# One ScalarE queue, two neighbouring steps exchanged: the rounding of an earlier unit ahead of the arctangent

## The chip, the cores and the metric

The kernel runs on one core of one Trainium2 chip. The metric is the device time of one execution in microseconds. Three runs of the kernel before gave 1058.86 to 1060.13 us, with a median of 1059.6 us.

## The reference

Three things are computed one after the other, all in float32. The first is a gated linear attention over 4 batches of 8 heads, 768 tokens and 48 values a head. Its output, regrouped to 3072 tokens of 384 features, goes through a first feed-forward stage with 2048 hidden units and the Mish function, and the result goes through a second one with 1536 hidden units and a sigmoid gate.

```python
def _attn_ref(q, k, v, f_logit):
    f = 1.0 / (1.0 + np.exp(-f_logit))
    for t in range(S):
        state = f[:, :, t, :, None] * state + np.einsum('bhd,bhe->bhde', k[:, :, t], v[:, :, t])
        y[:, :, t] = np.einsum('bhd,bhde->bhe', q[:, :, t], state)

def _moe_ref(x, w_in, w_out):
    h = x @ w_in
    sp = np.where(h > 20.0, h, np.log1p(np.exp(np.minimum(h, 20.0))))
    return (h * np.tanh(sp)) @ w_out

def _moe2_ref(x, w_gate, w_val, w_out):
    gate = 1.0 / (1.0 + np.exp(-(x @ w_gate)))
    return (gate * (x @ w_val)) @ w_out
```

## The kernel before, in words

The program has three stages. Attention runs from 0 to about 189.6 us of the span, the first feed-forward stage (Mish) from there to about 605 us, and the second one to the end. Each engine has its own hand-written queue, and semaphores join them. An engine works its queue strictly in the written order. The change is in the Mish stage alone, so the rest of this section is about it.

The 3072 tokens are taken in three passes (NPASS) of 1024 tokens. A pass is two tiles (TP) of 512 tokens. The 2048 hidden units are 16 blocks of 128. A **unit** i of a pass is one block with one tile, so a pass has N1 = 32 units, i = 0 to 31. A pass takes 33 steps (POS1), one per unit and an empty one at its end, because three buffer sets (NSET) are used in turn.

All matmuls are float32 products in three parts (high times high, high times low, low times high), which is what the helper `three` issues. So each matrix that feeds one is split into a rounded high part and a remainder.

For unit i the work is this, with the name of the function, the line and the engine:

- `hidden` (L841 to L843, TensorE): nine matmuls of 512 columns give the hidden values h(i) in one of two PSUM banks.
- `start` (L472, ScalarE): tanh of h/2.
- `silu` (L695, VectorE): a product with h, which also frees the PSUM bank.
- `angle` (L478, ScalarE): arctangent of the tanh. It waits on `tanh_done`.
- `square` (L484) and `shifted` (L490), ScalarE: two Square activations, each waiting for the one before it.
- `cubic` (L701) and `finish` (L708), VectorE: two products that end the Mish value g(i).
- `high` (L495, ScalarE): rounds g(i) to the high part `ghi`. It waits on `g_done`, which `finish` sets, and on `acc_done`, for a free buffer.
- `low` (L713, VectorE): the remainder `glo`.
- `project` (L841 to L843 with `ghi` and `glo`, TensorE): nine matmuls that add the unit to the sums in PSUM. It waits on `g_ready`, which `low` sets.

The queues are skewed against one another. In step i TensorE does `hidden` of unit i and then `project` of unit i-2 (LOOK = 2). ScalarE does `start`, `angle`, `square` and `shifted` of unit i and `high` of unit i-1. VectorE does `silu` of unit i, `low` of unit i-1, then `cubic` and `finish` of unit i. In the empty step TensorE has `project` of unit 30 straight behind that of unit 29, and ScalarE has only `high` of unit 31. In the first two steps of the next pass the sums are read out of PSUM: `sums_high` (L502, ScalarE, three copies) and `sums_low` (L721, VectorE, three subtractions).

GpSimd splits weights (L364 a cast, L366 a subtraction, both on 128x384 tiles). In the third pass it splits the weights of the next stage into the space of those just used: after `project` of every second unit it has two weight units to split, so four instructions in a row.

Of the kernel before, what the change touches and what calls it, by code (L numbers as in the profile page):

```python
# [81 lines left out]
def attention_mlp_mlp(nc, q, k, f, v, w_in, w_out1, w_gate, w_val, w_out2, out):  # L82
    with ExitStack() as ctx:
# [126 lines left out]
        def lag_b(p, i, lag):  # L210
            at = back(p, i, lag, POS1, NPASS)
            return at if at and at[1] < N1 else None
# [181 lines left out]
        def _(act):  # L394
# [102 lines left out]
            def sums_high(p, i):  # L497

                t = i - (N1 - TP)
                act.wait_ge(acc_done, p * N1 + i + 1)  # L500
                for c in range(KC):
                    act.activation(xhi[:, c, bass.ds(p * PASS + t * TILE, TILE)], acc[t * KC + c][:, :],  # L502
                                   ACT.Copy).then_inc(x2hi_done, 1)

            def mish(p, i):
                if (at := lag_b(p, i, LOOK + 1)) and at[1] >= N1 - TP:
                    sums_high(*at)
                for lag, do in ((0, start), (0, angle), (1, high), (0, square), (0, shifted)):
                    if at := lag_b(p, i, lag):
                        do(*at)  # L510

            run(act, NPASS, POS1, LOOK + 1, LOOK + 1, mish)


# [436 lines left out]
```

## Time and profile before

| what | value |
|---|---|
| median of three runs | 1059.6 us |
| the profiled execution | 1059.6 us, with a span of 1057.6 us |
| TensorE matmul, busy | 1015.0 us (96%) |
| TensorE weight load, busy | 824.8 us (78%) |
| VectorE, busy | 552.2 us (52%) |
| ScalarE, busy | 541.1 us (51%) |
| GpSimd, busy | 132.3 us (13%) |
| mean granted TensorE clock | 0.993 of 2.4 GHz |
| chain that ended last, by engine | PE 81%, DVE 10%, issue 5%, ACT 3% |

In the profile PE is TensorE, PEld its weight loads, DVE VectorE, ACT ScalarE and POOL GpSimd. Busy time is a share of the whole span. The Mish stage takes about 415 us of it, with 192 groups of nine matmuls on TensorE. A matmul's record is longer than the distance to the next one, since they are pipelined: the distance between two starts is what counts. An idle time is the gap on an engine just before an instruction, with the name of what ended it.

### The profile page before, as it was taken

What the parts mean: (1) busy time and instruction counts of PE and PEld (TensorE: products, weight loads), DVE (VectorE), ACT (ScalarE), POOL (GpSimd) and SP (SyncE); (2) the same over time, 40 slices, a digit from 0 to 9 for tenths busy, and PEclk for the clock granted to TensorE, in tenths of its full rate; (3) what the DMA queues carried; (4) which work ended last, traced back from release to release, by engine and by line L of the source; (5) the groups of instructions that cost most, each with busy time, mean ns of one, the idle gap of its engine ahead of it and who ended that gap; (6) DMA issues with size and microseconds to landing.
All of it is one profiled execution on the core that took longest, in us unless ns stands there. A gap on an engine that the chain in (4) does not pass through costs nothing.

```text
span 1057.6 us, 14107 instructions
## 1 busy us (share of the span) xinstructions
PE 1015.0 (96%) x4765; PEld 824.8 (78%) x4765; DVE 552.2 (52%) x843; ACT 541.1 (51%) x969; POOL 132.3 (13%) x147
## 2 busy tenths in 40 slices
PE   4999999899999999999999899999999999999997
PEld 3777777688887888878888688888888888888885
DVE  6999998566667666667777622222222222222221
ACT  5677776577777777787777622121321122321212
POOL 2222212500000000004455420000000000000000
PEclk9999999899999999999999999999999999999999
DMA  5444442200000000001111100000100000100001
GB/s 149 143 140 132 140 138 78 60 1 1 1 1 1 0 0 0 0 0 43 48 45 46 46 22 2 0 1 1 60 0 0 0 0 0 60 0 1 1 1 60
DMA packets 35339, 37.54 MB, mean 35 GB/s; under 512 B 4064, under 2 KB 26080, under 8 KB 35296
## 3 DMA queue, kind: packets, MB, share of 16 engines
q1 hardware_dynamic: 35296, 36.98, 11.7%
q8 instruction: 25, 0.41, 0.2%
q14 instruction: 18, 0.15, 0.0%
HBM read 32.24 MB, written 4.72 MB: 35 GB/s over the span
## 4 chain that ended last, share of the span: by engine, by line
PE 81%; DVE 10%; issue 5%; ACT 3%; DVEq 0%; DMA 0%; SPq 0%; ACTq 0%
PE bank L841 26%; PE bank L843 26%; PE bank L842 26%; DVE prefix L576 2%; DVE probs L603 1%; ACT qt L412 1%; DVE suffix L578 1%; DVE state L620 1%; DVE xlo L627 1%; PE bank L784 1%; PE bank L761 1%; DVE state L614 1%; DVE kb L592 1%; DVE qb L589 1%; PE bank L779 1%
## 5 line engine op out<-in xcount | busy, mean ns | idle before, releaser
L841 PE MATMUL bank<-xhi,whi 128*128 (+1 forms) x720 | 285.0, 396 | 4.2 <-DVE xlo L721 2.6
L843 PE MATMUL bank<-xhi,wlo 128*128 (+1 forms) x720 | 283.7, 394 | 0.0
L842 PE MATMUL bank<-xlo,whi 128*128 (+1 forms) x720 | 281.0, 390 | 0.0
L841 PE MATMUL bank<-ghi,whi 128*128 128x512 f32 x504 | 200.4, 398 | 8.1 <-DVE glo L713 7.8
L741 DVE TENSOR_TENSOR prod<-prod,bank 128x512 f32<-128x512 f32 x72 | 49.5, 688 | 290.2 <-PE bank L843 290.2
L843 PE MATMUL bank<-ghi,wlo 128*128 128x512 f32 x504 | 198.2, 393 | 0.0
L842 PE MATMUL bank<-glo,whi 128*128 128x512 f32 x504 | 197.0, 391 | 0.0
L841 PEld LDWEIGHTS bank<-xhi,whi 128*128 128x128 f32 x720 | 135.5, 188 | 33.6 <-DVE xlo L721 3.0
L843 PEld LDWEIGHTS bank<-xhi,wlo 128*128 128x128 f32 x720 | 135.4, 188 | 32.3
L842 PEld LDWEIGHTS bank<-xlo,whi 128*128 128x128 f32 x720 | 135.7, 188 | 31.0
L521 ACT ACTIVATE prod<-bank 128x512 f32<-128x512 f32 x72 | 43.2, 600 | 188.0 <-PE bank L843 188.0
L526 ACT ACTIVATE ghi<-prod 128x512 fp32r<-128x512 f32 x72 | 45.5, 632 | 155.4 <-DVE prod L741 155.4
L841 PEld LDWEIGHTS bank<-ghi,whi 128*128 128x128 f32 x504 | 95.0, 189 | 31.7 <-issue 6.5
L843 PEld LDWEIGHTS bank<-ghi,wlo 128*128 128x128 f32 x504 | 95.0, 188 | 22.7
L842 PEld LDWEIGHTS bank<-glo,whi 128*128 128x128 f32 x504 | 95.1, 189 | 21.1
L701 DVE SCALAR_TENSOR_TENSOR sets<-sets 128x512 f32<-128x512 f32 x96 | 77.5, 807 | 64.8 <-ACT sets L490 64.6
L472 ACT ACTIVATE sets<-bank 128x512 f32<-128x512 f32 x96 | 57.4, 598 | 82.6 <-PE bank L843 82.6
L713 DVE TENSOR_TENSOR glo<-sets,ghi 128x512 fp32r<-128x512 f32 x96 | 67.1, 699 | 45.0 <-ACT ghi L495 43.2
L412 ACT ACTIVATE qt<-qb,rtotal 64x128 f32<-64x128 f32 x192 | 76.6, 399 | 21.2 <-DVE rtotal L587 14.7
L761 PE MATMUL bank<-qt,kb 128*128 128x256 f32 x192 | 64.8, 436 | 23.2 <-ACT qt L412 15.4
L364 POOL CAST whi<-raw 128x384 fp32r<-128x384 f32 x44 | 36.3, 825 | 350.4 <-PE bank L843 336.6
L743 DVE TENSOR_TENSOR glo<-prod,ghi 128x512 fp32r<-128x512 f32 x72 | 50.8, 705 | 50.8 <-ACT ghi L526 50.8
(70 smaller groups left out, 1060.3 us busy)
## 6 DMA issues: line engine op xcount, KB each, us to landing
raw<-w_out_dram SPq DMA_DIRECT2D x28, 192.0 KB, 2.4
xb<-f_dram SPq DMA_DIRECT2D x48, 96.0 KB, 2.4
kb<-k_dram SPq DMA_DIRECT2D x48, 96.0 KB, 2.2
qb<-q_dram SPq DMA_DIRECT2D x48, 96.0 KB, 2.2
vb<-v_dram SPq DMA_DIRECT2D x24, 192.0 KB, 2.4
out_dram<-rows_out SPq DMA_DIRECT2D x18, 256.0 KB, 2.2
raw<-w_in_dram SPq DMA_DIRECT2D x16, 192.0 KB, 2.6
raw<-w_gate_dram SPq DMA_DIRECT2D x12, 192.0 KB, 2.5
```

The lines of the kernel that those rows point to most:

```text
L412: ins = act.activation(qt[rows, a, par, :], qb[rows, n % NCH, a, :], ACT.Copy, scale=rtotal[rows, n % 2, a:a + 1])
L472: act.activation(st[:, 0], h_ps[i % 2][:, :], ACT.Tanh, scale=0.5).then_inc(tanh_done, 1)
L521: act.activation(prod[:, i % NSET], h_ps[0][:, :], ACT.Sigmoid).then_inc(sig_done, 1)
L526: act.activation(ghi[:, i % 2], prod[:, i % NSET], ACT.Copy).then_inc(phi_done, 1)
L701: dve.scalar_tensor_tensor(st[:, 3], st[:, 3], Z_SHIFT, st[:, 2], ALU.add, ALU.mult).then_inc(cubic_done, 1)
L713: dve.tensor_tensor(glo[:, i % 2], sets[:, i % NSET, 1], ghi[:, i % 2].bitcast(F32), ALU.subtract).then_inc(g_ready, 1)
L741: dve.tensor_tensor(prod[:, i % NSET], prod[:, i % NSET], h_ps[1][:, :], ALU.mult).then_inc(p_done, 1)
L743: dve.tensor_tensor(glo[:, i % 2], prod[:, i % NSET], ghi[:, i % 2].bitcast(F32), ALU.subtract).then_inc(p_ready, 1)
L761: mm = pe.matmul(s_ps[a // 2][:, (a % 2) * 2 * C:(a % 2 + 1) * 2 * C], kb[:, n % 3, a, :], qt[:, a, :, :].rearrange("p h t -> p (h t)"), s ...
L841: pe.matmul(ps, hi, xh, start=first, stop=False)
L842: pe.matmul(ps, hi, xl, start=False, stop=False)
L843: return pe.matmul(ps, lo, xh, start=False, stop=last)
```

## The change

The order of five steps in ScalarE's queue is altered. `high` of the unit before stood behind `angle` of the present unit; now it stands ahead of it, right behind `start`. No instruction is added or removed, and no wait is altered. The queues of the other engines are the same.

```diff
@@ -505,7 +505,7 @@
             def mish(p, i):
                 if (at := lag_b(p, i, LOOK + 1)) and at[1] >= N1 - TP:
                     sums_high(*at)
-                for lag, do in ((0, start), (0, angle), (1, high), (0, square), (0, shifted)):
+                for lag, do in ((0, start), (1, high), (0, angle), (0, square), (0, shifted)):
                     if at := lag_b(p, i, lag):
                         do(*at)
```

On ScalarE in the middle of a pass, the queue from the last step of one unit into the next unit and the one after it was this before (`sets` are the three buffer sets, `bank` is PSUM with the hidden values, and `ghi` takes the rounded value of the unit before):

```order
L490 ACTIVATE sets<-sets,consts 128x512
L472 ACTIVATE sets<-bank 128x512
L478 ACTIVATE sets<-sets,consts 128x512
L495 ACTIVATE ghi<-sets 128x512
L484 ACTIVATE sets<-sets,consts 128x512
L490 ACTIVATE sets<-sets,consts 128x512
L472 ACTIVATE sets<-bank 128x512
L478 ACTIVATE sets<-sets,consts 128x512
```

At the same place on ScalarE it is now this:

```order
L490 ACTIVATE sets<-sets,consts 128x512
L472 ACTIVATE sets<-bank 128x512
L495 ACTIVATE ghi<-sets 128x512
L478 ACTIVATE sets<-sets,consts 128x512
L484 ACTIVATE sets<-sets,consts 128x512
L490 ACTIVATE sets<-sets,consts 128x512
L472 ACTIVATE sets<-bank 128x512
L495 ACTIVATE ghi<-sets 128x512
```

L495 has moved up by one row, so L478, L484 and L490 of the present unit all stand behind it now, where only L484 and L490 did.

The second place is ScalarE at the end of a pass, with unit 31, the empty step and the first copy of the sums. Before (the numbers tell PSUM banks and tensors apart; ISA is a wait):

```order
L472 ACTIVATE sets_75<-bank7 128x512
L478 ACTIVATE sets_75<-sets_75,consts_54 128x512
L495 ACTIVATE ghi_73<-sets_75 128x512
L484 ACTIVATE sets_75<-sets_75,consts_54 128x512
L490 ACTIVATE sets_75<-sets_75,consts_54 128x512
L495 ACTIVATE ghi_73<-sets_75 128x512
L502 ISA
L502 ACTIVATE xhi_51<-bank0 128x512
```

And now, on ScalarE at the same end of a pass:

```order
L472 ACTIVATE sets_75<-bank7 128x512
L495 ACTIVATE ghi_73<-sets_75 128x512
L478 ACTIVATE sets_75<-sets_75,consts_54 128x512
L484 ACTIVATE sets_75<-sets_75,consts_54 128x512
L490 ACTIVATE sets_75<-sets_75,consts_54 128x512
L495 ACTIVATE ghi_73<-sets_75 128x512
L502 ISA
L502 ACTIVATE xhi_51<-bank0 128x512
```

The first L495 is that of unit 30 and the second that of unit 31. Two instructions stood between them, and now three do.

## Rows read from the trace of the kernel before

**Rows 1.** Waits of all engines: waiting < waited for, us in total, times, longest.

```profile
DVE sets L701 <- ACT sets L490: 64.6, 92, 1.6
...
ACT sets L472 <- PE bank L843: 82.6, 90, 4.9
...
ACT ghi L495 <- DVE sets L708: 8.4, 7, 2.3
PE bank L841 <- DVE glo L713: 7.8, 6, 2.7
```

**Rows 2.** Timeline of a middle step: start us, duration us, instruction, idle before.

```profile
314.21 0.60 ACT L472 ACTIVATE sets<-bank 128x512 f32<-128x512 f32 x1 [0.90 <-PE bank L843]
...
314.85 0.73 ACT L478 ACTIVATE sets<-sets,consts 128x512 f32<-128x512 f32 x1
...
315.48 0.61 ACT L495 ACTIVATE ghi<-sets 128x512 fp32r<-128x512 f32 x1
...
316.00 0.71 ACT L484 ACTIVATE sets<-sets,consts 128x512 f32<-128x512 f32 x1
...
316.74 0.72 ACT L490 ACTIVATE sets<-sets,consts 128x512 f32<-128x512 f32 x1
...
317.50 0.69 DVE L701 SCALAR_TENSOR_TENSOR sets<-sets 128x512 f32<-128x512 f32 x1 [0.68 <-ACT sets L490]
...
318.16 0.40 PE L841 MATMUL bank<-ghi,whi 128*128 128x512 f32 x1
...
318.29 0.69 DVE L708 SCALAR_TENSOR_TENSOR sets<-sets 128x512 f32<-128x512 f32 x1
318.36 0.60 ACT L472 ACTIVATE sets<-bank 128x512 f32<-128x512 f32 x1 [0.90 <-PE bank L843]
```

**Rows 3.** Timeline at the end of the first pass, units 30 and 31.

```profile
323.77 0.61 ACT L495 ACTIVATE ghi<-sets 128x512 fp32r<-128x512 f32 x1
...
324.42 0.69 DVE L713 TENSOR_TENSOR glo<-sets,ghi 128x512 fp32r<-128x512 f32 x1 [0.59 <-ACT ghi L495]
...
325.16 0.50 PE L841 MATMUL bank<-ghi,whi 128*128 128x512 f32 x1 [0.62 <-DVE glo L713]
...
326.58 0.69 DVE L708 SCALAR_TENSOR_TENSOR sets<-sets 128x512 f32<-128x512 f32 x1
...
327.31 0.63 ACT L495 ACTIVATE ghi<-sets 128x512 fp32r<-128x512 f32 x1 [1.56 <-DVE sets L708]
```

**Rows 4.** Timeline of ScalarE, first unit of the third pass.

```profile
465.34 0.60 ACT L472 ACTIVATE sets<-bank 128x512 f32<-128x512 f32 x1 [0.28 <-PE bank L843]
465.97 0.72 ACT L478 ACTIVATE sets<-sets,consts 128x512 f32<-128x512 f32 x1
466.73 0.72 ACT L484 ACTIVATE sets<-sets,consts 128x512 f32<-128x512 f32 x1
```

**Rows 5.** Timeline: `high` early in each pass, `project` of unit 30.

```profile
203.21 0.63 ACT L495 ACTIVATE ghi<-sets 128x512 fp32r<-128x512 f32 x1 [1.08 <-DVE sets L708]
...
343.11 0.63 ACT L495 ACTIVATE ghi<-sets 128x512 fp32r<-128x512 f32 x1
...
460.82 0.50 PE L841 MATMUL bank<-ghi,whi 128*128 128x512 f32 x1 [0.62 <-DVE glo L713]
...
478.74 0.63 ACT L495 ACTIVATE ghi<-sets 128x512 fp32r<-128x512 f32 x1
...
596.53 0.47 PE L841 MATMUL bank<-ghi,whi 128*128 128x512 f32 x1 [0.72 <-DVE glo L713]
```

**Rows 6.** Timeline of the third pass, VectorE beside GpSimd.

```profile
588.54 1.02 POOL L366 TENSOR_TENSOR wlo<-raw,whi 128x384 fp32r<-128x384 f32 x1
...
588.78 1.33 DVE L701 SCALAR_TENSOR_TENSOR sets<-sets 128x512 f32<-128x512 f32 x1 [0.68 <-ACT sets L490]
...
590.21 0.81 DVE L708 SCALAR_TENSOR_TENSOR sets<-sets 128x512 f32<-128x512 f32 x1
```

**Rows 7.** Windows: stretch, busy us of each engine (instructions), granted clock, DMA.

```profile
200.00:204.00 4.00, 3.59 (x9) 2.89 (x10) 3.14 (x5) 2.86 (x6) 3.84 (x4) 0.57 0.34 98
```

## The prediction

> **What bounds the kernel now.** I read the waits first, then the timeline of one middle step, then the ends of the passes. In the middle of a pass TensorE waits for nothing: one step takes 318.36 - 314.21 = 4.15 us [rows 2], which is 18 matmuls at 0.23 us. ScalarE waits about 0.90 us for it in each step [rows 1, 2]. TensorE waits for the Mish value only 6 times in the whole stage, 7.8 us in total [rows 1], among them 0.62, 0.62 and 0.72 us ahead of `project` of unit 30 in the three passes [rows 3, 5]. So TensorE sets the pace, and the other engines have slack. The question is whether they still have it after the change.
>
> The number that decides this is not ScalarE's busy time (about 3.4 us of work in 4.15). It is a loop: `finish` of unit i-1 releases `high` of unit i-1. Whatever stands behind `high` in ScalarE's queue and leads to `finish` of unit i is in a chain that feeds itself once per unit. If one turn of it takes over 4.15 us, it, and not TensorE, sets the pace.
>
> **The loop before.** Each link is a distance between two starts:
> - `high` to `square`: 316.00 - 315.48 = 0.52 us [rows 2]
> - `square` to `shifted`: 316.74 - 316.00 = 0.74 [rows 2]
> - `shifted` to `cubic`: 317.50 - 316.74 = 0.76 [rows 2]
> - `cubic` to `finish`: 318.29 - 317.50 = 0.79, with rounding 0.80 in other steps; I take 0.80 [rows 2]
> - `finish` to the next `high`, where `high` is waiting: 327.31 - 326.58 = 0.73 [rows 3]
>
> The sum is 3.55 us, and the trace has it as such once, where TensorE does not hold it: 327.31 - 323.77 = 3.54 [rows 3]. That is 0.60 us under TensorE's 4.15, so the loop is hidden.
>
> **The loop after.** `angle` joins it. `high` to `angle` takes 0.52 us; the trace before has `high` ahead of `square` only, but neither follower depends on `high`, so I take the same value. `angle` to `square` is now bare, since nothing stands between them: 466.73 - 465.97 = 0.76 where that was so already [rows 4], against the 1.15 us that spanned a `high` before. I take 0.75, the 0.72 of the instruction and 0.03 for the semaphore. The turn is 0.52 + 0.75 + 0.74 + 0.76 + 0.80 + 0.73 = 4.30 us. The bounds of the new link are 0.52 + 0.63 (if `square` could follow without the wait's gap, as `angle` is followed by `high` now) and 0.63 + 0.76 (if `angle` followed `high` as `high` follows `angle` now), so 4.18 to 4.42 us for a turn. All are above 4.15. `start` is not in the loop: it is issued while VectorE does `cubic` and `finish`, which take 0.76 + 0.80 + 0.73 = 2.29 us from `shifted`, and `start` needs 0.63 + 0.51 of them. `silu` and `low` fit into the rest of VectorE's turn.
>
> **How it spends the slack.** At first `high` comes earlier: in that middle step 0.66 us after `start` (318.29 + 0.73 - 318.36) and not 1.27 [rows 2]. From `high` to its `project` it takes 325.16 - 323.77 = 1.39 us [rows 3]. In the middle step the value was there at 315.48 + 1.39 = 316.87, and `project` began at 318.16 [rows 2], so 1.29 us of slack. A loss of 0.15 us per unit eats this and the early gain in 9 to 13 units. From there each `project` waits, and at unit 30, which has no `hidden` ahead of it, the wait is about 2.1 us in place of 0.6. So the end of a pass follows from counting turns:
>
> - **First pass.** `high` of unit 1 is at 203.21 [rows 5], and by the new loop no sooner. 29 turns later, plus 1.39, `project` of unit 30 starts at 203.21 + 124.70 + 1.39 = 329.30. Before: 325.16 [rows 3]. That is +4.14 us.
> - **Second pass.** The first units are held by VectorE's `sums_low`, which the change leaves alone; `high` of unit 2 at 343.11 [rows 5] keeps its place in the pass. 343.11 + 28 x 4.30 + 1.39 = 464.90 against 460.82 [rows 5]: +4.08 us.
> - **Third pass, without GpSimd.** 478.74 + 120.40 + 1.39 = 600.53 against 596.53 [rows 5]: +4.00 us.
> - **GpSimd in the third pass.** Its splits of the next stage's weights run beside this. A `cubic` that begins inside L366 takes 1.33 us and not 0.69, and the `finish` behind it 0.81 [rows 6]. Before, that fell into the slack of 0.60 us of the loop. Now there is none and it adds in full. There are 14 such bursts from unit 1 to unit 27. The bursts start behind `project` of an odd unit, some 3.8 us after its `high` (1.39, then nine matmuls and the release), and last about 4.2 us, so with the new turn the `cubic` of the second unit after it, at 4.30 + 2.77 us, meets the last L366. Bounds: 0, if the new phase misses them; 0.64 + 0.12 + about a quarter more, so 1.0 us each, if a whole L366 is waited for. I take 0.64, the row's value for one caught `cubic`: 14 x 0.64 = +9.0 us.
> - **Between passes, twice.** `high` of unit 31 comes one new turn after that of unit 30, 4.30 and not 3.54 us. ScalarE had 0.28 us to spare ahead of `start` of the next unit 0 [rows 4]; the rest, 0.48, moves the next pass: +0.9 us for two. The end of the third pass is covered: TensorE does the first eighteen matmuls of the next stage there.
>
> Attention and the last stage do not move. Nothing in the queues of DMA, VectorE and TensorE is reordered; the stores and loads follow their consumers.
>
> Sum: 4.1 + 4.1 + 4.0 + 9.0 + 0.9 = 22.1 us. The profiled execution took 1059.6 us (its span 1057.6, 2.0 us around it), which is also the median, so the forecast is 1082 us, +2.1%.
>
> On the GpSimd term there is a rule. The row shows `cubic` begun 0.24 us after the start of a 1.02 us L366 and lengthened by 0.64 us [rows 6]. The Trainium skill (SBUF — State Buffer, "SBUF: two separate sides") says that VectorE and GpSimd share a pair of ports as an exclusive lock; a VectorE instruction with two SBUF inputs, against a GpSimd one that reads SBUF, blocks for the whole of the other. By that rule the loss depends on where in L366 the operation falls, and rises to a full L366, about 1.0 us, at the worst phase; the sum would be 14 x 1.0 = 14 us for this term and 1087 us in all. The trace agrees with the lock (588.54 + 1.02 = 589.56, and the 1.33 us end 0.55 us after it), and it speaks against this change, since a longer loop is exposed to every such block.
>
> **The rivals.**
> 1. *The loop misses GpSimd's bursts.* For: the phase of VectorE against `project` changes. Against: a burst takes some 4.2 us of every two turns, so a VectorE operation of the loop can hardly avoid it. 4.1 + 4.1 + 4.0 + 0.9 = 13.1 us: 1072.7 us.
> 2. *The bursts catch more*, two operations or a whole L366 each: 14 us, in all 27 us: 1087 us.
> 3. *Not slower: the earlier `high` is all that is seen.* The place is the wait ahead of `project` of unit 30. If the new turn takes under 4.15 us, nothing accumulates, and `high` of unit 30 is earlier by up to 1.27 - 0.66 = 0.61 us, so three waits of 0.62, 0.62 and 0.72 us shrink to almost nothing: -1.8 us, 1057.8 us. It decides from the point where `angle` and `square` together take under 1.12 us behind `high`, against my 1.27. Against it is that the second depends on the first, whose record alone is 0.72 us.
> 4. *The clock falls.* From 200 to 204 us, behind the one wait of 2.7 us [rows 1], the granted clock is 0.57, near the lower of its two levels, 1.2 and 2.4 GHz [rows 7]. The new waits of about 2.1 us at unit 30 could do so again. Nine matmuls fill 3.6 us of that stretch in place of 9 x 0.23 = 2.1, so 1.5 us each for up to three, and three more at unit 0: +9 us, 1091 us.
>
> **How the numbers follow.** Forecast 62% (own range 1077 to 1085), rival 1 15%, rival 2 12%, rival 4 5%, rival 3 6%. The range that holds 8 in 10 runs from 1071, which takes in rival 1, to 1087, rival 2. Within 0.2% (2.1 us) is what measurement cannot tell from no change. Slower by more is all but rival 3: 94%. Rival 3 is mostly within the bound: 4% same, 2% faster.
>
> **What the profile after would show.** In the middle of a pass from unit 13 on, `high` to `high` and `project` to `project` are 4.30 us apart and not 4.15, in the third pass 4.6 on average. `high` waits for `finish` in nearly every step, so L495 behind L708 rises from 7 waits to about 90 and to some 80 us, while ScalarE's 82.6 us of waiting for TensorE at L472 mostly go. TensorE's waits behind L713 become some 60, and about 2 us at unit 30. The third pass is longer by 13 us or so, the other two by 4 to 5. If the step stays at 4.15 us, the loop is wrong; if the third pass grows like the others, the GpSimd term is; if the matmul distance rises above 0.23 us, it is the clock.

## The result

| | before | after |
|---|---|---|
| median | 1059.87 us (1058.86 to 1060.62, 4 runs) | 1086.32 us (1085.74 to 1086.52, 4 runs) |
| profiled execution | 1059.6 us, span 1057.6 | 1084.98 us, span 1083.0 |

The ratio is 1.0249, with a 95% interval of 1.0231 to 1.0267: slower by 2.5%, where 2.1% was forecast (1082 us, range 1071 to 1087).

The waits of the profile after, in the columns of [rows 1], and next to the lines that stood there:

```profile
DVE sets L701 <- ACT sets L490: 123.7, 92, 1.6
ACT ghi L495 <- DVE sets L708: 109.1, 94, 2.1
...
PE bank L841 <- DVE glo L713: 19.1, 20, 2.6
...
ACT sets L472 <- PE bank L843: 8.1, 7, 5.4
```

The relation has turned round. ScalarE waited 82.6 us for TensorE before and waits 8.1 us now; `high` waited for `finish` 7 times and does so 94 times out of 96, for 109.1 us. ScalarE and VectorE have become a ring of two engines waiting for each other, at 50% and 51% busy. Busy shares alone would not name them as the bound. The chain that ended last says it in one line (share of the span by engine; before it was PE 81%, DVE 10%, ACT 3%):

```profile
PE 46%; ACT 25%; DVE 21%; issue 6%; DVEq 1%; DMA 0%; SPq 0%; ACTq 0%
```

One turn of the ring in the middle of the first pass, on ScalarE, in the timeline after (start, duration, idle before):

```profile
315.56 0.63 ACT L495 ACTIVATE ghi<-sets 128x512 fp32r<-128x512 f32 x1 [1.07 <-DVE sets L708]
316.10 0.71 ACT L478 ACTIVATE sets<-sets,consts 128x512 f32<-128x512 f32 x1
316.84 0.72 ACT L484 ACTIVATE sets<-sets,consts 128x512 f32<-128x512 f32 x1
317.60 0.72 ACT L490 ACTIVATE sets<-sets,consts 128x512 f32<-128x512 f32 x1
318.23 0.58 ACT L472 ACTIVATE sets<-bank 128x512 f32<-128x512 f32 x1
319.88 0.63 ACT L495 ACTIVATE ghi<-sets 128x512 fp32r<-128x512 f32 x1 [1.07 <-DVE sets L708]
```

and its two links on VectorE:

```profile
318.36 0.69 DVE L701 SCALAR_TENSOR_TENSOR sets<-sets 128x512 f32<-128x512 f32 x1 [1.44 <-ACT sets L490]
319.15 0.69 DVE L708 SCALAR_TENSOR_TENSOR sets<-sets 128x512 f32<-128x512 f32 x1
```

319.88 - 315.56 = 4.32 us a turn, against TensorE's 4.15 [rows 2]. The links are 0.54, 0.74, 0.76, 0.76, 0.79 and 0.73. `start` (L472) stands in the hole ahead of `high` and costs nothing, as reckoned.

TensorE now takes its pace from the ring. `project` follows `hidden` at 0.33 and 0.31 us where two matmuls are 0.23 us apart otherwise, and one `project` starts 4.32 us behind the other (312.75 and 317.07 us):

```profile
312.42 0.39 PE L843 MATMUL bank<-xhi,wlo 128*128 x1
312.75 0.47 PE L841 MATMUL bank<-ghi,whi 128*128 128x512 f32 x1
313.06 0.40 PE L842 MATMUL bank<-glo,whi 128*128 128x512 f32 x1
```

Such a hold is shorter than the overlap of two matmul records, so the list of waits leaves it out: of TensorE's 20 waits for `low` none lies in the middle of the first two passes.

In the third pass GpSimd's splits come beside it. VectorE, then GpSimd, after:

```profile
500.16 1.31 DVE L713 TENSOR_TENSOR glo<-sets,ghi 128x512 fp32r<-128x512 f32 x1
502.29 1.19 DVE L701 SCALAR_TENSOR_TENSOR sets<-sets 128x512 f32<-128x512 f32 x1 [0.82 <-ACT sets L490]
503.59 0.69 DVE L708 SCALAR_TENSOR_TENSOR sets<-sets 128x512 f32<-128x512 f32 x1
```

```profile
499.91 1.02 POOL L366 TENSOR_TENSOR wlo<-raw,whi 128x384 fp32r<-128x384 f32 x1
500.87 0.97 POOL L364 CAST whi<-raw 128x384 fp32r<-128x384 f32 x1
501.92 1.02 POOL L366 TENSOR_TENSOR wlo<-raw,whi 128x384 fp32r<-128x384 f32 x1
```

`cubic` (L701) begins inside the second L366 and takes 1.19 us, not 0.69. 501.92 + 1.02 = 502.94, and `cubic` ends 0.54 us behind that. Every second turn is 4.82 us, the others 4.32.

Where the 25.4 us between the two profiled executions are, from the starts of `high` (L495) of units 2 and 30 in each pass (the Mish stage ends at 607.67 us before and 633.01 after, where TensorE's first matmul of the last stage starts):

| stretch | before | after | difference | forecast |
|---|---|---|---|---|
| start to `high` 30, first pass | 323.77 | 328.50 | +4.73 | +4.14 |
| to `high` 2, second pass | 19.34 | 19.69 | +0.35 | +0.48 |
| to `high` 30, second pass | 116.32 | 120.80 | +4.48 | +4.08 |
| to `high` 2, third pass | 19.31 | 20.91 | +1.60 | +0.48 |
| to `high` 30, third pass | 116.31 | 128.29 | +11.98 | +4.0 + 9.0 |
| to the end of the Mish stage | 12.62 | 14.82 | +2.20 | 0 |
| the last stage | 449.93 | 449.99 | +0.06 | 0 |

The first row holds the attention stage too. The change leaves that alone, but it ended 0.76 us earlier in the execution after (the first matmul of the Mish stage starts at 188.89 us, before at 189.65). Counted from there, the first pass is longer by 5.49 us and not by 4.73.

The two stretches to `high` 2 of the third pass and to the end of the Mish stage, both well over the forecast, hold something else. Behind the wait of unit 30, TensorE's matmuls are 0.43 us apart and not 0.23 for about eight in a row. The first matmul behind the wait in the third pass, and three of the eight:

```profile
620.29 0.47 PE L841 MATMUL bank<-ghi,whi 128*128 128x512 f32 x1 [2.59 <-DVE glo L713]
...
622.14 0.63 PE L842 MATMUL bank<-glo,whi 128*128 128x512 f32 x1
622.57 0.63 PE L843 MATMUL bank<-ghi,wlo 128*128 128x512 f32 x1
623.00 0.63 PE L841 MATMUL bank<-xhi,whi 128*128 128x512 f32 x1
```

The granted clock of this stretch and of the one in the second pass is 0.72 over six microseconds (windows, columns as in [rows 7]), that is, for part of it the lower of the two levels of 1.2 and 2.4 GHz:

```profile
471.00:477.00 6.00, 6.00 (x21) 4.77 (x20) 2.08 (x3) 3.31 (x6) 0.00 (x0) 0.72 0.00 0
621.00:627.00 6.00, 6.00 (x20) 4.72 (x20) 4.33 (x6) 2.09 (x4) 0.59 (x1) 0.72 0.22 60
```

Eight times 0.2 us is 1.6 us, less where other engines hold the end anyway. In the first pass the same wait (1.90 us) was followed by no such stretch. And `low` of unit 30 in the third pass took 1.29 us beside GpSimd, which is the other 0.6 us of the +2.20.

### The profile page after: what moved, and what is told of

The parts are those of the page before. It is cut to its first block, busy times and chain, and to the rows that moved or that the text cites. A ratio compares the mean times of both kernels' runs of the same rounds, so it can differ in the third digit from the quotient of the medians.

```text
span 1083.0 us, 14107 instructions
## 1 busy us (share of the span) xinstructions
PE 1028.8 (95%) x4765; PEld 820.5 (76%) x4765; DVE 551.1 (51%) x843; ACT 539.8 (50%) x969; POOL 123.0 (11%) x147
## 4 chain that ended last, share of the span: by engine, by line
PE 46%; ACT 25%; DVE 21%; issue 6%; DVEq 1%; DMA 0%; SPq 0%; ACTq 0%
PE bank L841 14%; PE bank L843 14%; PE bank L842 14%; DVE sets L701 7%; ACT sets L484 6%; ACT sets L490 6%; DVE sets L708 6%; ACT sets L478 5%; ACT ghi L495 5%; DVE prefix L576 2%; DVE probs L603 1%; ACT qt L412 1%; PE bank L784 1%; PE bank L761 1%; DVE state L620 1%
## 5 line engine op out<-in xcount | busy, mean ns | idle before, releaser
L841 PE MATMUL bank<-ghi,whi 128*128 128x512 f32 x504 | 205.4, 408 | 19.4 <-DVE glo L713 19.1
L701 DVE SCALAR_TENSOR_TENSOR sets<-sets 128x512 f32<-128x512 f32 x96 | 74.6, 777 | 123.9 <-ACT sets L490 123.7
L495 ACT ACTIVATE ghi<-sets 128x512 fp32r<-128x512 f32 x96 | 60.8, 633 | 109.1 <-DVE sets L708 109.1
L713 DVE TENSOR_TENSOR glo<-sets,ghi 128x512 fp32r<-128x512 f32 x96 | 75.1, 782 | 11.1 <-ACT ghi L495 2.1
L364 POOL CAST whi<-raw 128x384 fp32r<-128x384 f32 x44 | 33.7, 765 | 383.8 <-PE bank L843 370.0
```

The costliest lines, as they stand in the source:

```text
L495: act.activation(ghi[:, i % 2], sets[:, i % NSET, 1], ACT.Copy).then_inc(ghi_done, 1)
L701: dve.scalar_tensor_tensor(st[:, 3], st[:, 3], Z_SHIFT, st[:, 2], ALU.add, ALU.mult).then_inc(cubic_done, 1)
L713: dve.tensor_tensor(glo[:, i % 2], sets[:, i % NSET, 1], ghi[:, i % 2].bitcast(F32), ALU.subtract).then_inc(g_ready, 1)
L841: pe.matmul(ps, hi, xh, start=first, stop=False)
```

## The experiments

The theory on trial is the loop: the ring from `high` to the next `high` sets the pace once a turn is longer than TensorE's 4.15 us, and GpSimd adds to it. The rivals are that the time goes to TensorE's restarts behind the many new waits (the first distance is 0.31 and not 0.23 us) and to its clock, and that GpSimd is not what lengthens the third pass. All ratios are against the kernel before on the same chip, whose median was 1059.9 to 1061.1 us there. The changed kernel was not measured again beside the experiments, so a difference between its median and that of an experiment is uncertain by about 1 us. The last column is the distance from `high` of unit 2 to that of unit 30 in the three passes, in the timeline. Edits of the order of the steps are shown against the kernel before, and "..." marks what is left out of an edit.

| run | median us | ratio, 95% interval | unit 2 to 30, us |
|---|---|---|---|
| before | 1059.87 | | 116.05, 116.32, 116.31 |
| after | 1086.32 | 1.0249 (1.0231 to 1.0267) | 120.79, 120.80, 128.29 |
| high_first | 1138.27 | 1.0719 (1.0687 to 1.0750) | 138.44, 138.43, 138.94 |
| new_cubic_384 | 1073.13 | 1.0118 (1.0094 to 1.0143) | 117.04, 117.08, 124.90 |
| new_cubic_256 | 1058.38 | 0.9974 (0.9958 to 0.9991) | 116.02, 115.81, 115.99 |
| old_cubic_256 | 1059.31 | 0.9984 (0.9968 to 0.9999) | 116.04, 116.26, 116.38 |
| new_thin_split | 1076.85 | 1.0142 (1.0114 to 1.0169) | 120.78, 120.80, 120.81 |
| old_thin_split | 1059.45 | 0.9992 (0.9978 to 1.0006) | 116.04, 116.32, 116.30 |
| filler | 1085.53 | 1.0238 (1.0213 to 1.0263) | 120.78, 120.78, 128.25 |
| early_at_end | 1060.56 | 1.0000 (0.9987 to 1.0013) | 115.44, 115.70, 115.88 |
| ends_moved | 1061.60 | 1.0012 (0.9998 to 1.0026) | 115.62, 115.72, 115.87 |
| high_after_square | 1064.07 | 1.0028 (1.0013 to 1.0042) | 116.07, 116.14, 116.21 |
| high_last | 1089.89 | 1.0263 (1.0228 to 1.0298) | 121.71, 121.72, 123.45 |

### A longer loop

```diff
-                for lag, do in ((0, start), (0, angle), (1, high), (0, square), (0, shifted)):
+                for lag, do in ((1, high), (0, start), (0, angle), (0, square), (0, shifted)):
```

> The rounding `high` of unit i-1 stands one place further forward still, ahead of `start` of unit i; nothing is left out. Loop theory: `start` joins the chain from `high` to the next `high`, which adds its 0.63 us link; the turn of 4.315 us becomes about 4.95 us, 85 turns x 0.63 = +54 us on the changed kernel, so about 1140 us, and `high` to `high` 4.95 us apart in the first two passes. Rival (the loss is what TensorE pays to restart behind a wait, 0.1 us each, and for its clock): the number of waits is the same, one a unit, so about 1086 us, as the changed kernel. A rival by which an earlier rounding helps would have it faster than 1086.

Measured: 1138.27 us, for 1140 expected. ScalarE's timeline:

```profile
259.72 0.63 ACT L495 ACTIVATE ghi<-sets 128x512 fp32r<-128x512 f32 x1 [1.55 <-DVE sets L708]
260.25 0.58 ACT L472 ACTIVATE sets<-bank 128x512 f32<-128x512 f32 x1
260.87 0.72 ACT L478 ACTIVATE sets<-sets,consts 128x512 f32<-128x512 f32 x1
...
264.66 0.63 ACT L495 ACTIVATE ghi<-sets 128x512 fp32r<-128x512 f32 x1 [1.55 <-DVE sets L708]
```

A turn is 4.94 us: one more instruction between `high` and `high` has added its 0.62 us. The restart theory has no room for this. The profile lists 90 waits of TensorE for `low` here and 20 after the change, where the short ones are not listed; even 70 more at 0.1 us would be 7 us and not 52. The third pass has hardly any of GpSimd's loss (138.94 against 138.43), so how much the bursts catch depends on the phase. Here most of a burst falls where VectorE waits: the `low` inside it takes 0.85 us, and `cubic` and `finish` keep their 0.69 (564.93 to 568.08 us). The forecast's first rival, wrong for the changed kernel, is right for this one.

### A shorter loop, in two doses, and a control

```diff
-                dve.scalar_tensor_tensor(st[:, 3], st[:, 3], Z_SHIFT, st[:, 2], ...)
+                dve.scalar_tensor_tensor(st[:, 3, 0:256], st[:, 3, 0:256], Z_SHIFT, st[:, 2, 0:256], ...)
```

> The new order, with the first product on VectorE (`cubic`) done on 256 of the 512 columns (the other half keeps its old values). Loop theory: this link shortens by 0.27 us, the turn is 4.05 us and below TensorE's 4.15, so in the first two passes the distance between two `high` is 4.15 us again and the loss there goes; the third pass has about 0.5 us per pair of turns from GpSimd and loses perhaps 2 us. 1058 to 1063 us. Rival (restart and clock of TensorE, or ScalarE's own queue being too full): nothing is taken from TensorE or ScalarE, so 1083 to 1086 us.

> The order before, with the same halved `cubic`: the control. Loop theory: the loop is 3.55 us there and hidden, so taking 0.27 us out of it gives at most 0.27 us at each of the three waits ahead of `project` of unit 30: 1059 us, -0.8 us. If it became faster by several us, the halved product would explain the run with the new order by itself.

Measured: 1058.38 us with the new order and 1059.31 us with the old one. TensorE sets the pace again:

```profile
263.44 0.60 ACT L472 ACTIVATE sets<-bank 128x512 f32<-128x512 f32 x1 [0.90 <-PE bank L843]
263.93 0.62 ACT L495 ACTIVATE ghi<-sets 128x512 fp32r<-128x512 f32 x1
...
267.59 0.60 ACT L472 ACTIVATE sets<-bank 128x512 f32<-128x512 f32 x1 [0.90 <-PE bank L843]
```

With 0.27 us taken out of one VectorE instruction, on an engine that is 51% busy, 28 us of kernel time are back. `high` does not wait here (23 times and 11.9 us in the whole stage, for 94 and 109.1), and the idle time of 0.90 us ahead of `start` is that of [rows 2]. The same cut under the old order is worth 0.2%. So nothing is wrong with the new order as such: it needs a turn below 4.15 us. The third pass did not lose the 2 us expected: two turns take 4.05 + 4.24 = 8.29 us there beside GpSimd, which is two steps of TensorE.

The second dose is 384 columns in place of 256:

> The new order, with `cubic` on 384 of the 512 columns (the rest keeps its old values). Loop theory: the turn is 4.315 - 0.133 = 4.18 us, 0.04 over TensorE's 4.145, so in the first two passes 28 turns lose 1.0 us, less than the slack that the early rounding brings, and only the waits at unit 30 grow a little; in the third pass GpSimd's 0.5 us per pair of turns adds 7 us less the slack of 1.9. About 1065 us. A cost in proportion to what is left of the product would be half way between the changed kernel and the run with 256 columns, 1072 us.

Measured: 1073.13 us, a miss by 8 us. The turn was as expected, 4.18 us, with 4.69 + 4.18 for a pair in the third pass, so 0.51 us from GpSimd. What was wrong is "less the slack of 1.9". The slack in the middle of a pass is real, but the pass ends with unit 30, whose `project` was already waiting for `high` before. There, all delay of `high` counts in full: +0.99, +0.76 and +8.59 us from unit 2 to unit 30 in the three passes. Of the 13.4 us between the profiled executions these are 10.3; 2.3 more stand behind unit 30 of the third pass, where again eight matmuls are 0.43 us apart, and 0.9 ahead of unit 2 of the first, of which 0.5 are the attention stage's.

The median of 1073 us is nearer to the 1072 us of the rival, a cost in proportion to what is left of the product, than to the 1065 us of the loop theory. The total alone would speak for the rival. What decides against it is where the time is: the first two passes lost 4.74 and 4.48 us with the full `cubic`, 0.99 and 0.76 with 384 columns and nothing with 256, as 28 turns of 4.32, 4.18 and 4.15 us give it, and not half; the third pass lost 11.98, 8.59 and nothing. That the sum comes out near half way is chance.

### GpSimd's work taken away, and a control

```diff
-                    split(SLOTS + n, whi[:, n, :], wlo[:, n, :])
+                    thin(SLOTS + n, whi[:, n, 0:8], wlo[:, n, 0:8])
```

`thin` is `split` with the same waits and two instructions, on 8 columns.

> The new order, with GpSimd's 32 weight units of the third pass split on 8 of 384 columns (so the second stage works with wrong weights), which takes GpSimd's work away from beside VectorE and leaves the waits. Loop theory: the third pass becomes like the second, 120.8 us from `high` of unit 2 to that of unit 30 and not 128.3, and the 1.3 us `low` ahead of the last wait is 0.7: -8 us, 1078 us. Rival (GpSimd is not the cause of the longer third pass; TensorE's waits or clock are): under 2 us, 1085 us.

> The order before, with GpSimd's 32 weight units of the third pass split on 8 of 384 columns (wrong weights in the second stage): the control. Loop theory: GpSimd's blocks fell into slack, so at most the 0.1 us by which unit 30 waits longer in the third pass: 1059.5 to 1060 us. If it were 5 us or more faster, GpSimd's cost would have been there before the change too.

Measured: 1076.85 us, 9.5 us less than the changed kernel, and 1059.45 us for the control, the same as before. In the profiled executions the Mish stage is 9.4 us shorter than after the change: 7.5 between units 2 and 30 of the third pass, 0.6 behind them, and 1.2 that are not GpSimd's, because the stretch of slow matmuls behind the second pass is missing in this execution. A burst is short now,

```profile
542.04 0.44 POOL L372 CAST whi<-raw 128x8 fp32r<-128x8 f32 x1 [7.48 <-PE bank L851]
542.56 0.20 POOL L374 TENSOR_TENSOR wlo<-raw,whi 128x8 fp32r<-128x8 f32 x1
```

and the third pass is the same as the second, 120.81 us. GpSimd's share of the loss is shown, and that it was free before the change.

### Does TensorE's clock fall because of the wait?

```diff
                 pe.wait_ge(w_ready, 2 * j + 2)
+                if i == N1 - 2:
+                    pe.wait_ge(silu_done, p * N1 + i + 1)
+                    for c in range(2 * KC):
+                        pe.matmul(h_ps[i % 2][:, :], whi[:, 2 * j, 0:P], xhi[:, 0, ...], start=True, stop=True)
```

> The new order, with six matmuls of 512 columns more, whose result is overwritten, ahead of `project` of unit 30 in each pass, in the place where TensorE waits 1.9 to 2.6 us (they take 1.4 us). If the stretches of matmuls at 0.43 us behind those waits in the second and third pass come from the wait, they go, at eight x 0.2 = 1.6 us for the third and 1.2 for the second: 1083.5 us, -2.8 us. If the clock falls for another cause, the time stays at 1086.3 and the stretches stay.

Measured: 1085.53 us, 0.8 us less than the changed kernel and inside the spread of both. In the profile the stretches behind unit 30 are gone: the granted clock from 471 to 477 and from 620 to 627 us is 1.00. But a new one stands at the start of the next stage, behind the wait of 2.6 us that all kernels have there:

```profile
471.00:477.00 6.00, 5.51 (x25) 3.94 (x23) 3.60 (x6) 4.11 (x7) 0.00 (x0) 1.00 0.00 0
620.00:627.00 7.00, 5.88 (x26) 4.79 (x26) 5.37 (x7) 3.98 (x7) 2.54 (x3) 1.00 0.21 56
632.00:637.00 5.00, 4.65 (x13) 3.72 (x14) 2.30 (x3) 1.23 (x2) 4.76 (x7) 0.66 0.43 121
```

This is inconclusive. The stretch behind the second pass is also missing in `new_thin_split`, which has no such matmuls and the same wait (1.91 us), so that it is gone here proves nothing; and one profile of each kernel is too little for something that comes and goes at the same place. What the traces do show is its price: from `high` of unit 30 to that of unit 2 into the third pass it is 19.68 us in `filler` and in `new_thin_split`, and 20.91 us after the change.

### Can the earlier rounding be had where it does not accumulate?

```diff
+                early = ((0, start), (1, high), (0, angle), (0, square), (0, shifted))
+                late = ((0, start), (0, angle), (1, high), (0, square), (0, shifted))
-                for lag, do in ((0, start), (0, angle), (1, high), (0, square), (0, shifted)):
+                for lag, do in early if i == N1 - 1 else late:
```

> The order before in every step but one: only in the step of unit 31 does `high` (of unit 30) stand ahead of `angle`. Loop theory: one turn of 4.3 us per pass does not accumulate, and the waits ahead of `project` of unit 30 of 0.62, 0.62 and 0.72 us go to under 0.1: -1.8 us, 1058.1 us. Rival (the early rounding is bad wherever it stands): 1060 or more.

Measured: 1060.56 us, ratio 1.0000, so a gain of 1.8 us did not show. The wait ahead of `project` of unit 30 is gone in the first two passes, as expected. But `high` of unit 31 now comes 4.32 us behind that of unit 30 and not 3.54, so all that follows it at the end of the pass (the sums, `start` of the next unit 0) kept most of its time, and the next wait of TensorE, ahead of `project` of unit 0, grew from the 1.56 us of before to this (the line numbers are two higher in this kernel):

```profile
338.85 0.50 PE L843 MATMUL bank<-ghi,whi 128*128 128x512 f32 x1 [1.75 <-DVE glo L715]
```

From `high` of unit 30 to that of unit 30 a pass later it is 135.39 us against 135.66, and then 135.57 against 135.62: of the 0.6 us at a pass's end 0.27 and 0.05 remain, and only the last pass keeps all. In the profiled executions the Mish stage is 417.1 us long against 418.0, so half of the gain is there, and seven matmuls at 0.43 us behind it, which the execution before does not have, cost more than that. Against an interval of 1.4 us to either side, 0.9 us cannot be told from nothing.

The last version works on the waits at unit 0 as well:

```diff
-                for lag, do in ((0, start), (0, angle), (1, high), (0, square), (0, shifted)):
+                for lag, do in early if i in (1, N1 - 1) else late:
...
+                sums = (at := lag_b(p, i, LOOK + 1)) and at[1] >= N1 - TP
...
-                for lag, do in ((0, silu), (1, low), (0, cubic), (0, finish)):
+                steps = ((1, low), (0, silu), (0, cubic), (0, finish)) if i == 1 else ((0, silu), (1, low), (0, cubic), (0, finish))
+                for lag, do in steps:
+                    if do is cubic and sums and i == 0:
+                        sums_low(*lag_b(p, i, LOOK + 1))
```

> The order before in the middle of a pass; in the step of unit 31 and of unit 1 `high` stands ahead of `angle`, on VectorE `low` of unit 0 ahead of `silu` of unit 1, and the first subtraction of the sums (`sums_low`) ahead of `cubic` of unit 0. Loop theory: as with unit 31 alone, -1.8 us, and the two waits of 1.54 us ahead of `project` of unit 0 shrink to some 0.4: -2.3 us; in all -4 us, 1056 us. Rival: the waits at unit 0 are held by something behind, and it stays at 1058.

Measured: 1061.60 us, ratio 1.0012 (0.9998 to 1.0026): no gain, against the 4 us expected. Without the stretches of slow matmuls the Mish stage is 414.3 us long, against 414.8 before and 413.9 in `early_at_end`, so the three further moves brought nothing more. The wait ahead of `project` of unit 0 went down to 0.44 us, and a new one of 1.34 us stands ahead of that of unit 1:

```profile
471.62 0.50 PE L847 MATMUL bank<-ghi,whi 128*128 128x512 f32 x1 [0.44 <-DVE glo L715]
...
477.38 0.47 PE L847 MATMUL bank<-ghi,whi 128*128 128x512 f32 x1 [1.34 <-DVE glo L715]
```

The wait was handed on, not removed. What may take the time at a pass's start is the reading out of the sums, six copies and six subtractions beside the first units; no run tests this.

### The other side: `high` later

`high` between `square` and `shifted`:

> `high` stands one place later than in the kernel before, between `square` and `shifted`; nothing is left out. Loop theory: the loop is 0.52 + 0.76 + 0.80 + 0.73 = 2.8 us and hidden, and the rounding itself is 0.74 us later, which the 1.29 us of slack in the middle of a pass still covers; only the waits ahead of `project` of unit 30 grow by 0.74 each: +2.2 us, 1062.4 us.

Measured: 1064.07 us, +3.8 us, for +2.2 expected. The middle of the passes is unchanged (116.1 us), so the loss is at the ends alone. In the profiled execution the Mish stage is 421.5 us long against 418.0, and the distances between matmuls that are near 0.43 us hold 4.3 us over 0.23 each in it, against 3.2 us before. Without them it is 417.2 against 414.8, so +2.4 us, with the waits ahead of `project` of unit 30 at 1.38, 1.38 and 1.47 us for 0.62, 0.62 and 0.72. The other 1.1 us of the stage are the slow matmuls. (The Mish stage before, from 189.65 to 607.67 us, is 418.0 us long; the 415 us given ahead of the prediction were a rough figure.)

`high` behind `shifted`:

> `high` stands last in the step, behind `shifted`; nothing is left out. The loop from `high` to `high` is gone, but the rounding is 1.48 us later than before and the slack was 1.29, so another loop closes, through TensorE and over two units: from the end of `hidden` of unit i to `start` 0.20, to `high` of unit i-1 0.63 + 0.75 + 0.74 + 0.63 = 2.75, to its `project` 1.39, together 4.34 us; `hidden` of unit i+2 ends 4.25 us behind that `project`. Two units then take 8.59 us, 4.30 each, in all three passes, since `cubic` and GpSimd are not in this loop: 0.15 us x 90 = +13 us, 1073 us. If only the position behind `angle` mattered it would be 1060 to 1062.

Measured: 1089.89 us, +29.6 us, where 13 were expected. The second loop is there: in the first two passes two turns take 4.56 + 4.14 us in alternation, 4.35 each, and ScalarE waits for TensorE and TensorE for VectorE in turn. The waits of this kernel:

```profile
ACT sets L472 <- PE bank L843: 95.3, 89, 5.4
PE bank L841 <- DVE glo L713: 20.5, 31, 3.0
```

Of the 29.6 us, 18.2 are between units 2 and 30 (121.71, 121.72 and 123.45 us against 116.05, 116.32 and 116.31). The expected turn of 4.30 us was 0.05 short, which is 4 us in all. In the third pass the long turn is 4.66 us beside GpSimd, which the expectation had held to be outside this loop: 1.7 us. And it left out that the same order also delays the first units of each pass: 7.9 us ahead of unit 2 in the three. The last 3.6 us are behind the third pass (1.5), in the last stage, which starts with eight slow matmuls (1.7), and in the attention stage of this execution (0.4).

## Why the prediction was right, and where it was off

The direction and most of the size came from the cause that was forecast, a ring above TensorE's pace. But 1086.32 us lies beyond the forecast's own range of 1077 to 1085, 0.7 us from the upper bound of 1087 and nearer to the figure of rival 2 than to 1082. Rival 2 is not what happened: the bursts caught less than forecast, not more. The forecast was short by other terms, and part of them cancelled. Between the profiled executions (25.4 us for 22.1) the largest are +2.9 us for the slow matmuls, +1.3 for the turn, +0.6 for `low` of unit 30 and -1.5 for the bursts.

- **The mechanism and its place.** The loop from `high` to `high` with `angle` in it, 4.30 us against 4.15, is shown: the trace has the turn, `high_first` makes it longer and `new_cubic_256` makes it vanish, with prices near those reckoned from the turn (1138.27 us for 1140, 1058.38 for 1058 to 1063). The price in `new_cubic_384` was not (1073 us for 1065), though the turn was.
- **The turn** was 4.315 us on average and not 4.30. `high` to `angle` took 0.54 and not 0.52 us. 85 turns by 0.015 are 1.3 us.
- **The first pass** was +4.73 and not +4.14. GpSimd caught `cubic` and `finish` of unit 1, for 0.99 us together (that turn took 5.29 us), which the forecast put at no change. `high` of unit 0 was 0.8 us earlier and hid most of it, and that was luck: the attention stage had ended 0.76 us earlier in this execution. From the start of the Mish stage the pass was longer by 5.49 us, and the term was 1.35 us too small.
- **GpSimd in the third pass** was forecast at 9.0 us, from 0.64 us for each of 14. It was 0.50 us for most of them and 0.97 for the first: 128.29 - 120.80 = 7.5 us. With 0.6 us at `low` of unit 30, for which no term stood, 8.1 us. The taking away of GpSimd's work gave 9.4 us in the profile, of which 1.2 are the clock's.
- **Between passes** 0.35 us were measured where the clock kept up (0.48 forecast), 1.60 where it did not.
- **The signs.** `high` to `high` at 4.32 us, 94 waits for `finish` and the two kinds of pass came as forecast. `high` waited 109.1 us for `finish` and not some 80. TensorE's listed waits behind `low` are 20 and not some 60: six at the starts of the passes and at unit 30 of the first two, and fourteen further on in the third; the holds of 0.1 us in the middle of the others fall under the overlap of the records.
- **The clock**, rival 4 with 5%, was no rival but an addition: two stretches in the profiled execution, up to 1.6 us each, for which the sum had nothing. It had been priced as an alternative to the loop when it could only come on top, since it is the loop that makes the waits at unit 30. With 1.3 us from the turn it is most of what the forecast was short by. Why it came behind two of these three waits is open.
- **"It spends the slack first"** was right for the middle of a pass but counted nowhere, and the sum rightly did not use it. The expectation for `new_cubic_384` did, and missed.
- **Rival 3**, the earlier rounding as a small gain: even where it does not accumulate only 0.9 us of 1.8 are in the profile and none in the median, because most of the wait moves to unit 0.

## What to carry to other kernels

Before moving an instruction in a queue, write down the ring it is in: from its own start, through everything behind it in its queue that leads to its own release one iteration later, each link read from the trace as a distance between starts. Compare the sum with the pace of the engine that bounds; being under it is free and being over it costs the difference in every iteration, whatever the busy shares say. A ring just under the pace has one more enemy: anything that lengthens a link now and then, here GpSimd's splits beside VectorE's products, was free as long as there was room and is paid in full when there is none. A move can also close another ring than the one it was checked for: `high` last in the step left this one and closed one through TensorE, at 29.6 us.

## What the runs showed that was not expected

- The stretches of about eight or fourteen matmuls at 0.43 us stand in different places in the profiles of nearly the same kernels: behind unit 30 in the second and third pass after the change, at the start of the next stage in `filler`, behind unit 30 of the third pass alone in `new_cubic_384` and `new_thin_split`. Beyond the first units of the Mish stage, those named here follow a wait of 1.9 us or more, but the same waits are also followed by none (1.90 us in the first pass after the change, 2.61 us at the start of the last stage before and after it). The wait of 2.6 us at the start of the last stage is in all thirteen profiles; seven have a stretch behind it and six have none. So a single profile can be 1.5 to 2.9 us longer for this alone. What decides is open.
- The earlier rounding was expected to be worth 0.6 us a pass at the end at least; of the first two, 0.27 and 0.05 us remained.
- VectorE's `low` was caught by GpSimd too (1.31 us in place of 0.69) and this cost nothing, since it is not in the ring, except once, at unit 30, where it is what TensorE waits for.
